# Attention with pooled queries on one NeuronCore: seven value bursts per pair in place of nine, the output transposes a period later

## The reference

```python
def _attn_ref(q, k, v):                       # 4 x 8 heads, seq 1152, head_dim 64
    q_pool = q.reshape(B, H, S // 2, 2, D).mean(axis=3)
    scores = scale * np.matmul(q_pool, k.transpose(0, 1, 3, 2))
    scores = scores - np.max(scores, axis=-1, keepdims=True)
    attn = np.exp(scores)
    attn = attn / (np.sum(attn, axis=-1, keepdims=True) + 1e-09)
    return np.matmul(attn, v)
```

## Time and profile before

| | us |
|---|---|
| median of 3 runs | 829.89 (825.88 to 831.99) |
| profiled execution | 830.63 |
| its span, first to last instruction | 828.6 |
| TensorE busy (matmuls) | 796.7 |
| VectorE busy | 502.6 |
| ScalarE busy | 466.8 |
| GpSimd busy | 174.6 |

### The profile page before, as it was taken

One profiled execution on the slowest core, in us unless ns is written; L12 is line 12 of the kernel. 1 busy time (PEld: TensorE's weight loads), 2 busy tenths in 40 slices (PEclk: granted clock), 3 DMA queues, 4 the chain that ended last, 5 costly groups with the idle time before them and its releaser, 6 DMA issues. The chain is left out here.

```text
span 828.6 us, 17284 instructions
## 1 busy us (share of the span) xinstructions
PE 796.7 (96%) x5747; PEld 603.5 (73%) x5747; DVE 502.6 (61%) x966; ACT 466.8 (56%) x896; POOL 174.6 (21%) x233
## 2 busy tenths in 40 slices
PE   4999999999999999999999999998999999999997
PEld 3777777777777777777777777763334788888875
DVE  6657666666566566665765766745124566666664
ACT  4766666766666667666676676642014453334342
POOL 3431422413314224133141340000000330000000
PEclk9999999999999999999999999999999799999999
DMA  7937365383473652834636518546999001010011
GB/s 247 269 88 181 74 150 118 90 192 85 114 171 73 155 114 85 199 83 117 156 81 162 113 30 226 223 152 266 380 393 384 5 1 51 0 52 14 39 51 26
DMA packets 83000, 112.03 MB, mean 135 GB/s; under 512 B 45328, under 2 KB 47376, under 8 KB 82448
## 3 DMA queue, kind: packets, MB, share of 16 engines
q1 hardware_dynamic: 82544, 110.91, 47.3%
q10 hardware_dynamic: 416, 0.59, 0.2%
HBM read 71.37 MB, written 4.72 MB: 92 GB/s over the span
## 5 line engine op out<-in xcount | busy, mean ns | idle before, releaser
L534 PE MATMUL scores<-k_stack,q_stack 128*128 128x384 f32 x960 | 274.5, 376 | 0.6 <-ACT probs L674 0.6
L479 PE MATMUL tbank<-ident,probs 128*128 128x128 f32 x1296 | 220.3, 279 | 4.3 <-DVE pt L816 2.5
L702 ACT COPY pt<-tbank 128x384 f32<-128x384 f32 x256 | 122.9, 480 | 144.1 <-PE tbank L479 142.9
L479 PEld LDWEIGHTS tbank<-ident,probs 128*128 128x128 f32 x1296 | 156.7, 140 | 61.1 <-issue 40.4
L674 ACT ACTIVATE probs<-scores,neg_max 128x1152 f32<-128x1152 f32 x144 | 176.0, 1222 | 8.1 <-PE tbank L479 2.1
L761 DVE TENSOR_REDUCE row_max<-scores 128x1 f32<-128x384 f32 x144 | 80.1, 556 | 129.3 <-PE scores L534 127.4
L569 PE MATMUL obank<-pt,v_in 128*64 128x256 f32 x1152 | 148.8, 389 | 0.0
L534 PEld LDWEIGHTS scores<-k_stack,q_stack 128*128 128x128 f32 x960 | 147.7, 191 | 1.2 <-ACT probs L674 1.0
L754 DVE TENSOR_REDUCE row_max<-scores 128x1 f32<-128x768 f32 x144 | 136.7, 949 | 4.0 <-PE scores L534 1.3
L569 PEld LDWEIGHTS obank<-pt,v_in 128*64 128x64 f32 x1152 | 72.8, 136 | 49.3 <-issue 23.5
L332 POOL TENSOR_TENSOR k_hi<-k_lo,one 128x512 fp32r<-128x512 f32 (+1 forms) x45 | 37.2, 826 | 297.9 <-ACT k_lo L619 277.0
(11 more groups left out here) (202 smaller groups left out, 768.3 us busy)
## 6 DMA issues: line engine op xcount, KB each, us to landing
weights<-in_moe_w SPq DMA_DIRECT2D x7, 2048.0 KB, 12.4
v_in<-in_v SPq DMA_DIRECT2D x16, 576.0 KB, 4.1
k_in<-in_k SPq DMA_DIRECT2D x30, 288.0 KB, 4.9
k_stack<-k_hi SPq DMA_DIRECT2D x30, 288.0 KB, 3.6
k_stack<-k_lo SPq DMA_DIRECT2D x30, 288.0 KB, 3.5
q_in<-in_q SPq DMA_DIRECT2D x15, 512.0 KB, 4.8
q_stack<-q_hi SPq DMA_DIRECT2D x30, 144.0 KB, 3.3
q_stack<-q_lo SPq DMA_DIRECT2D x30, 144.0 KB, 3.9
```

The costliest lines, as they stand in the source:

```text
L479: last = nc.tensor.transpose(tbank[:, bank, cols], src, ident[0:rows, 0:rows])
L534: last = nc.tensor.matmul(scores[:, bank, 0:CH], q_stack[at.par][:, h, order, cols], k_stack[at.par][:, h, keys], start=(x == 0), stop=(x ...
L702: nc.scalar.copy(pt_out(at, e), tbank[:, bank_of(at, e), 0:3 * P].rearrange("p (r q) -> p r q", r=3)).then_inc(out_by_act, 1)
```

## The change

The burst of group 0 in period 7 goes, its nine key tiles are split 3, 3, 3 over periods 6, 8 and 9 instead of 3, 2, 2, 2 over 6, 7, 8 and 9. The tail group's nine key tiles run in one burst in period 13 (period 4 of the next pair) instead of five there and four in period 14. O0 moves from period 5 to period 6 and O1 from 7 to 8.

```diff
-EXTRA = {(1, 1): "K0", (2, 1): "K1", (3, 1): "Q0", (4, 1): "KQ", (5, 1): "O0", (7, 1): "O1"}
+EXTRA = {(1, 1): "K0", (2, 1): "K1", (3, 1): "Q0", (4, 1): "KQ", (6, 1): "O0", (8, 1): "O1"}
...
-PV = {6: (0, (0, 1, 2)), 7: (0, (3, 4)), 8: (0, (5, 6)), 9: (0, (7, 8)),
+PV = {6: (0, (0, 1, 2)), 8: (0, (3, 4, 5)), 9: (0, (6, 7, 8)),
       10: (1, (0, 1, 2)), 11: (1, (3, 4, 5)), 12: (1, (6, 7, 8)),
-      13: (2, (0, 1, 2, 3, 4)), 14: (2, (5, 6, 7, 8))}
+      13: (2, tuple(range(NK)))}
```

## The result

The changed kernel takes 841.31 us (median of 4 runs, 839.98 to 843.93), the one before 828.14 in the runs beside it (median of 4): a ratio of 1.016, with a 95% interval of 1.0126 to 1.0193. It is 13.2 us slower; the forecast was 843.

What follows compares the result with a forecast made beforehand. The prediction took PE's own stream to bound the kernel. From 830.63 us, - 9.6 - 2.5 - 0.4 + 25.4 gave 843.5; the runs' median, 0.7 lower, made it 842.8, stated as 843, range 836 to 849.

Steps and rivals of the forecast that it cites:

- What bounds the kernel: Attention's steady part: PE's own stream sets the time; its only waits are 2.5 us in 480 us, for DVE's copy.
- The loop, 2.86 us: From one chunk in bank 2 to the next, through DVE and ACT; a period without burst can't be shorter.
- rival 2: No change: only one bare period waits, or each waits half; 830 to 832, or 835.5 with printed idle; chance 0.08.
- 31 more waits of 0.82: Period 5 of pairs 1 to 15 and period 7 of pairs 0 to 15 wait for exp: 25.4 us more.
- The check that gave 0.75: Pair 0, period 5: second estimate of the loss per wait, 1.05 less 0.30 between transpose and chunk: 0.75 us.
- 0.30 us for a burst, 9.6 in all: Entering and leaving a burst costs PE 0.30 us; two bursts fewer in 16 pairs save 9.6 us.
- The rival that followed from this alone, 818 us: Attention: fewer bursts are faster, with the loop hidden under other work; 818 us, chance 0.04.
- 2.5 us for DVE's late copy: Period 4: transposes wait 0.21 us for DVE's copy; a longer tail burst ahead of them saves 2.5 us.
- 0.4 us at the end of the attention: Before the last O1, PE's wait for the last group's copy goes: 0.4 us less, no more than 0.6.
- O0 in period 6 at nothing: PE pays O0's 0.43 us in period 6 instead of 5, with no wait for its bank: no net cost.
- The clock: The granted clock stays at 1.00 (2.4 GHz) despite the new waits: no effect on the time.
- the harsher case (waits before O0 or T(6,1)): Period 6: late exp pushes ACT's copies, 0.3 us more, 16 to 31 times; 848 to 853 us, chance 0.08.

Runs made afterwards that it cites:

- e6: Kernel before, with one more small VectorE operation ahead of neg_max in every tile: attention +1.81 us against before, ratio 1.0004.
- e8: Kernel before, with exp writing no row sums (they are set to 1 once): attention -1.18 us against before, ratio 0.9971.
- e7: Changed kernel, with exp writing no row sums (they are set to 1 once): attention +10.12 us against before, ratio 1.011.
- e9: Kernel before, with value matmuls of groups 0 and 1 at full width (128 columns of V, all 128 partitions): attention +88.83 us, ratio 1.106.
- e10: Kernel before, with VectorE's inverse row sums at the end of period 2 instead of 3: attention -3.43 us, ratio 0.9968.
- e1: Kernel before, with only the outputs moved (O0 to period 6, O1 to 8), nine bursts kept: attention +0.61 us, ratio 1.0021.
- e11: Kernel before, with the tail in one burst, O0 and O1 as period 5's extra jobs, group 2's copy at period 5: attention +4.48 us, ratio 1.006.
- e2: Kernel before, with only group 0 in three bursts (periods 6, 8, 9), tail and outputs unchanged: attention +6.90 us, ratio 1.0095.
- e3: Kernel before, with only the tail in one burst, outputs where they were: attention -1.51 us, ratio 0.9969.
- e4: Changed kernel, with O0 and O1 put back in periods 5 and 7: attention +5.24 us against before, ratio 1.0073.
- e12: Kernel before, with group 0 in three bursts (periods 6, 7, 9), O1 in period 8, inverses at the end of period 2: attention -7.11 us, ratio 0.9934.
- e5: Changed kernel, with one more small VectorE operation ahead of neg_max in every tile: attention +16.72 us against before, ratio 1.0196.

## Why the prediction was right

The time, 841.3 against 843, and the cause are those of the forecast. Of the 1.7 us between them nearly all is the base: the forecast started from 829.89 us for the kernel before, which took 828.14 beside the changed one. Point by point:

- **What bounds the kernel.** PE's own stream, with a loop close under it. e6 and e8 show the other side: before the change, 0.13 us more or 0.09 less in the loop reached PE only at the wait of period 4.
- **The loop, 2.86 us.** 2.84 in the changed kernel, 2.97 with a step added, 2.75 with one taken away. The single bare period of pair 0 gave it to 0.02 us. What I added up against rival 2, 2.78 us from the times of the parts, is no measure of it: parts overlap (of the read's 0.19 us only 0.09 count, e7), and the starts in a trace are what rules that rival out.
- **31 more waits of 0.82.** 32 waits stand in the profile, with pair 0's; each costs 2.84 - 2.04 = 0.80, or 24.8 us in all, where I had 25.4. The period after a wait is 0.04 us longer (4.11 for 4.07, 4.48 for 4.44), which brings it back to 26; no run shows what these 0.04 us are. Printed are 17.7 us, as said. The check that gave 0.75 took away the 0.30 us that lie between T(t,2) and its chunk behind a burst; with none there it is 0.24, and 1.05 - 0.24 = 0.81.
- **0.30 us for a burst, 9.6 in all.** e9 and the short transposes confirm price and cause: it goes with the change of tile size. The Trainium skill, "TensorEngine Tiling (Array Packing)", Key Properties, states that such a change drains TensorE; the trace agrees in that each change costs time, and doesn't show the drain itself. The rival that followed from this alone, 818 us, is excluded: the 9.6 us are less than half of what the waits cost.
- **2.5 us for DVE's late copy.** This term was too small. The 12 waits are gone, and e10, which takes away only them, gains 3.4: each cost 0.28 us and not the printed 0.21. The tail's burst of 36 took 1.20 us up to the next transpose, one of 16 took 0.62, so 16 more instructions cost 0.46 for my 0.49. Together they make period 4 3.60 us for my 3.68; periods 6 and 8 came out 0.04 longer each, and the steady pair at 34.09 for my 34.11.
- **0.4 us at the end of the attention.** This term failed. From the tail's burst to the next stage's DMA it took 553.73 - 550.40 = 3.33 us before and 567.19 - 563.92 = 3.27 after. The wait before O1 is gone, but DVE's normalisation of O0, which used to run under the second burst, now stands at the end. The gain is 0.06.
- **O0 in period 6 at nothing** held: period 6 is 4.11, no wait before it, and e1 costs 0.6 us in all.
- **The clock** stayed at 1.00 in 60 to 545 us of the changed kernel.
- **The sum.** -9.6 - 2.5 - 0.4 + 25.4 = +12.9, measured on the attention +13.04. With the terms as the runs gave them it is -9.6 - 3.4 - 0.1 + 26.0 = +12.9 again: three terms were off by 0.3 to 0.9 us and cancel, so that the sum came out within 0.2 us is luck. The rivals: no change (in its form of 835.5 us too) and faster are excluded by the interval; the harsher case (waits before O0 or T(6,1)) didn't occur here, but did in e11.

That the loss lies in the bare periods and not in the moved outputs or the longer bursts is shown by the halves: +0.61 (e1), +6.90 (e2), -1.51 (e3), and +5.24 with both halves and the outputs back (e4).

## What to carry to other kernels

Where a chain through other engines ties each round to the one before (here 2.84 us by way of maxima and exp), every period of the bounding engine has to be as long as the chain by itself: work taken out of a long period is saved, work taken out of a short one is not, and it is the shortest period after the change, not the mean, that has to be worked out. Fewer, larger bursts paid here only where the period stayed long enough (e12; the gain of e3 is that of a late copy), and the same transposes were nearly free in one period and cost their full time in another (e4 against the changed kernel). The beginning of the kernel, where the pipeline was still filling, showed a bare period, and the chain's length could be read there before any change; it is worth looking for one.

## What I had not expected of the hardware

- Value matmuls on half the array's columns, the two halves taken in turn, follow each other in 0.107 us, and the same moving columns at full width in 0.217 (e9).
- The price of a change of tile size, 0.30 us for a burst's entry and exit together, showed no part that any change of operands would cost: at full width it was nothing within 0.02 us (e9).
- Of two DVE steps in a row on single columns, 0.21 us each in the trace, the second adds only 0.13 (e5); the read of the accumulator, 0.19 us, adds 0.09 to the exp (e7).
